# Attention, top-2 experts and a gated layer in one kernel: GpSimd's weight parts, VectorE's routing and a table are placed anew in the attention loop

## The reference, cut to what matters

```python
# q, k, v: 2 batches x 8 heads x 768 x 64; 4 sink keys, window of 128
scores = q @ k.T / sqrt(D), kept where key < n_sink or 0 <= query - key < window
a = exp(scores - max); a = a / (sum(a) + 1e-9)
x = a @ v                                            # 1536 tokens x 512
logits = x @ w_gate + log1p(exp(x @ w_noise)) * noise  # 8 experts
top2, weights = the two largest logits and their softmax
for each expert e: out += weight * (relu(x[mask] @ w1[e]) @ w2[e])   # 512 -> 1024 -> 512
h = out @ w_in                                       # 512 -> 2048
g = h * tanh(log1p(exp(h)))
result = g @ w_out                                   # 2048 -> 512
```

## Time and profile before

| | before |
|---|---|
| median of the runs (3) | 784.29 us (783.91 to 784.30) |
| the profiled execution's own time | 783.87 us |
| its span, first to last instruction | 781.8 us |
| TensorE busy | 760.9 us, 97% |
| VectorE busy | 515.4 us, 66% |
| GpSimd busy | 314.2 us, 40% |
| ScalarE busy | 285.4 us, 37% |

### The profile page before, as it was taken

One profiled execution on the slowest core, in us unless ns is written; L12 is line 12 of the kernel. 1 busy time (PEld: TensorE's weight loads), 2 busy tenths in 40 slices (PEclk: granted clock), 3 DMA queues, 4 the chain that ended last, 5 costly groups with the idle time before them and its releaser, 6 DMA issues.

```text
span 781.8 us, 13281 instructions
## 1 busy us (share of the span) xinstructions
PE 760.9 (97%) x4228; PEld 627.1 (80%) x4229; DVE 515.4 (66%) x905; ACT 285.4 (37%) x594; POOL 314.2 (40%) x331
## 2 busy tenths in 40 slices
PE   8999969999999999999999999989999999999997
PEld 5888757888888888888888888768888888888886
DVE  6789965545445454544545445468998888878876
ACT  6888713030303003030030300356555554545443
POOL 5599936673833708337083918511020020000000
PEclk9999979999999999999999999999999999999999
DMA  6475574644532615417153624010000110010001
GB/s 208 159 252 177 158 235 138 200 161 136 187 123 75 222 38 180 128 64 231 41 176 119 200 96 122 29 54 29 28 27 28 55 54 1 1 54 1 1 0 55
DMA packets 49486, 82.87 MB, mean 106 GB/s; under 512 B 18080, under 2 KB 22240, under 8 KB 49440
## 3 DMA queue, kind: packets, MB, share of 16 engines
q10 hardware_dynamic: 13600, 33.96, 13.2%
q1 hardware_dynamic: 31440, 33.89, 13.1%
q0 software_dynamic: 4400, 14.42, 6.6%
HBM read 66.01 MB, written 16.25 MB: 105 GB/s over the span
## 4 chain that ended last, share of the span: by engine, by line
PE 87%; DVE 6%; issue 3%; ACT 2%; POOL 1%; another core or an unknown queue 1%; DMA 0%; DVEq 0%; ACTq 0%; POOLq 0%
PE bank L1345 21%; PE bank L1356 21%; PE bank L1420 16%; PE bank L1401 15%; PE bank L1329 4%; PE bank L1235 2%; PE bank L1322 2%; PE bank L1210 2%; PE bank L1219 1%; PE bank L1244 1%; PE bank L1194 1%; PE bank L1393 1%; DVE x_sb L887 0%; DMA xg<-x_dram,first_idx 0%
## 5 line engine op out<-in xcount | busy, mean ns | idle before, releaser
L577 POOL TENSOR_TENSOR wgt<-stage,wgt 128x1024 f32 (+1 forms) x64 | 151.2, 2402 | 101.2 <-ACT wgt L738 101.2
L1356 PE MATMUL bank<-wgt,hT 128*128 (+1 forms) x744 | 185.3, 398 | 0.0
L1345 PE MATMUL bank<-wgt,xT 128*128 (+1 forms) x744 | 182.6, 394 | 0.0
L1345 PEld LDWEIGHTS bank<-wgt,xT 128*128 128x128 f32 x744 | 137.3, 188 | 27.5 <-DVE xT L1039 0.2
L738 ACT ACTIVATE wgt<-stage 128x1024 f32 (+1 forms) x64 | 61.6, 1045 | 265.0 <-PE bank L1356 252.0
L1356 PEld LDWEIGHTS bank<-wgt,hT 128*128 128x128 f32 x744 | 135.2, 188 | 25.3
L1420 PE MATMUL bank<-wgt,gT 128*128 128x512 f32 x576 | 141.3, 395 | 4.8 <-DVE gT L1137 4.8
L1401 PE MATMUL bank<-x2T,wgt 128*128 128x512 f32 (+1 forms) x588 | 138.1, 385 | 0.9 <-DVE x2T L1114 0.9
L1420 PEld LDWEIGHTS bank<-wgt,gT 128*128 128x128 f32 x576 | 108.4, 190 | 28.7 <-DVE gT L1137 6.1
L1401 PEld LDWEIGHTS bank<-x2T,wgt 128*128 128x128 f32 x588 | 108.6, 188 | 23.0 <-POOL wgt L651 1.1
L1083 DVE TENSOR_SCALAR h<-bank 128x512 f32<-128x512 f32 x62 | 42.9, 692 | 60.7 <-PE bank L1345 56.5
(11 more groups left out here) (174 smaller groups left out, 935.5 us busy)
## 6 DMA issues: line engine op xcount, KB each, us to landing
stage<-in_moe_w ACTq DMA_DIRECT2D x48, 512.0 KB, 3.4
stage<-in_moe_w SPq DMA_DIRECT2D x16, 512.0 KB, 5.4
y_dram<-y_sb SPq DMA_DIRECT2D x31, 256.0 KB
stage<-in_moe_w_in ACTq DMA_DIRECT2D x8, 512.0 KB, 4.0
stage<-in_moe_w_out ACTq DMA_DIRECT2D x8, 512.0 KB, 4.1
v_in<-in_v SPq DMA_DIRECT2D x8, 384.0 KB
x_dram<-x_sb SPq DMA_DIRECT2D x16, 192.0 KB, 2.7
out<-o_sb SPq DMA_DIRECT2D x12, 256.0 KB, 2.0
```

Of the source, the lines that this page charges most:

```text
L577: nc.gpsimd.tensor_tensor(cols(parity, 1, u * UNIT, UNIT), stage[:, u, :], cols(parity, 0, u * UNIT, UNIT).bitcast(fp32), ALU.subtract).th ...
L1345: ins = T.matmul(HA[half][:], xT[:, a, c, :], cols(par, b, c * F + half * 512, 512), start=c == 0 and n == 0, stop=c == NC - 1 and n == 2)
L1356: ins = T.matmul(YB[kk % 2][:], hT[:, a, c, :], cols(par, b, NC * UNIT + c * DM, DM), start=c == 0 and n == 0, stop=c == F // P - 1 and n ...
```

## The change

GpSimd's weight parts start at attention unit 10 and take five units to a weight unit, in the first, second and fourth of them. The table is a quarter as wide, is made in the pass of unit 42, and its readers repeat it by broadcast. VectorE's routing of batch 0 is spread over the passes of units 34 to 46. SP loads two weight units right after q and k and before it waits for the value matmuls.

```diff
--- before.py
+++ after.py
@@ -112,7 +112,7 @@
     xT_att = [attn.tensor(f"xT_att{i}", [P, 2, P], fp32) for i in range(2)]
     assert attn.at <= attn_end, (attn.at, attn_end)
     hot = Region(wgt_at + 2 * WCOLS * 4)
-    ramps = hot.tensor("ramps", [P, P, 2 * NT], f16)
+    ramps = hot.tensor("ramps", [P, P, QT], f16)
     row_hot = [hot.tensor(f"row_hot{i}", [P, P, NT], f16) for i in range(2)]
     assert hot.at <= wgt_at + 2 * WCOLS * 4 + 4 * (2 * S + 2 * QT * SEC)
 
@@ -261,7 +261,7 @@
         probs_ready = sem("probs_ready")
         probs_transposed = sem("probs_transposed")
         pT_ready = sem("pT_ready")
-        WEIGHTS_FROM = 14
+        WEIGHTS_FROM, WEIGHT_UNITS, WEIGHT_PARTS = 10, 5, (0, 1, 3)
         pT_cut = sem("pT_cut")
         pv_ready = sem("pv_ready")
         xT_copied = sem("xT_copied")
@@ -436,13 +436,12 @@
                 if i + 1 < NP:
                     sp.wait_ge(qk_ready, 4 * i)
                     load_qk(i + 1, (i + 1) % 2)
+                for u in range(2 * (i - 2), min(2 * (i - 1), UNITS)):
+                    src, to = unit_of(0, u)
+                    sp.dma_start(to, src).then_inc(unit_loaded[u], 16)
                 sp.wait_ge(pv_ready, QT * (i - 1))
                 load_v(i, i % 2)
                 store_x(i - 2)
-
-                for u in range(2 * (i - 2), min(2 * (i - 1), UNITS)):
-                    src, to = unit_of(0, u)
-                    sp.dma_start(to, src).then_inc(unit_loaded[u], 16)
 
                 if i == NP - 1:
                     sp.wait_ge(consts_ready, 1)
@@ -564,11 +563,12 @@
                     cut_probs(n - 1)
                     pad_sums(n - 2)
                 for u in (n, n + 1):
-                    if u >= WEIGHTS_FROM and (u - WEIGHTS_FROM) // 4 < UNITS and (u - WEIGHTS_FROM) % 4 < 3:
-                        first_set((u - WEIGHTS_FROM) // 4, (u - WEIGHTS_FROM) % 4)
-                if n == PROBS - 2:
+                    unit, part = (u - WEIGHTS_FROM) // WEIGHT_UNITS, (u - WEIGHTS_FROM) % WEIGHT_UNITS
+                    if 0 <= unit < UNITS and part in WEIGHT_PARTS:
+                        first_set(unit, WEIGHT_PARTS.index(part))
+                if n == PROBS - QT:
                     pool.wait_ge(qk_ready, 4 * NP)
-                    nc.gpsimd.tensor_copy(ramps[:], ramp[:].unsqueeze(2).broadcast_to([P, P, 2 * NT])).then_inc(ramps_ready, 1)
+                    nc.gpsimd.tensor_copy(ramps[:], ramp[:].unsqueeze(2).broadcast_to([P, P, QT])).then_inc(ramps_ready, 1)
 
             def remainders(s, parity):
                 for u in range(UNITS):
@@ -967,7 +967,7 @@
                     dve.wait_ge(ramps_ready, 1)
                 for w in range(2):
                     ms = slice(w * NT + g * QT, w * NT + (g + 1) * QT)
-                    V.tensor_tensor(row_hot[w][:, :, js], ramps[:, :, ms], r_h[:, ms].unsqueeze(1).broadcast_to([P, P, QT]),
+                    V.tensor_tensor(row_hot[w][:, :, js], ramps[:], r_h[:, ms].unsqueeze(1).broadcast_to([P, P, QT]),
                                     ALU.is_equal).then_inc(rows_ready, 1)
 
             V = nc.vector
@@ -990,19 +990,22 @@
                     qk_remainder(i + 1, t - 1)
                 if u == PROBS - 3 * QT:
                     gate_sums(0, 0, QT).then_inc(sums_ready, 1)
+                if u == PROBS - 2 * QT - 2:
+                    noisy_gates(0)
                 if u == PROBS - 2 * QT:
-                    noisy_gates(0)
                     pick_max(0, 0, rt3["lg"][:, 0:QT])
+                if u == PROBS - 2 * QT + 2:
                     pick_first(0, 0)
+                if u == PROBS - QT - 2:
+                    hide_best(0)
                 if u == PROBS - QT:
-                    hide_best(0)
                     pick_max(0, 1, by_token("cut"))
+                if u == PROBS - QT + 2:
                     pick_first(0, 1)
-                if u == PROBS - QT + 2:
+                    count_rows(0)
                     score_gap(0)
-                    count_rows(0)
+                if u == PROBS - 2:
                     first_expert(0)
-                if u == PROBS - 2:
                     rank_rows(0)
                 if u >= 6:
                     norm_step(u - 6, 2)
@@ -1052,7 +1055,8 @@
             after(V.tensor_reduce(rt["begin"][:], sel, AX.X, ALU.add))
             V.scalar_tensor_tensor(rt["p01"][:], rt["begin"][:], float(P), rt["p01"][:], ALU.mult, ALU.add)
             after(V.tensor_tensor(a_h[:], rt["begin"][:], a_u[:], ALU.add))
-            after(V.tensor_tensor(slot_hot[:], ramps[:, 0:32], a_h[:].unsqueeze(1).broadcast_to([P, 32, M]), ALU.is_equal))
+            after(V.tensor_tensor(slot_hot[:].rearrange("p t (g j) -> p t g j", j=QT), ramps[:, 0:32].unsqueeze(2).broadcast_to([P, 32, M // QT, QT]),
+                                  a_h[:].rearrange("p (g j) -> p g j", j=QT).unsqueeze(1).broadcast_to([P, 32, M // QT, QT]), ALU.is_equal))
             V.tensor_tensor(slot_hot[:], slot_hot[:], tok_h[:].unsqueeze(1).broadcast_to([P, 32, M]), ALU.mult).then_inc(hots_ready, 1)
             split_xT(0)
             dve.wait_ge(idx_summed, 1)
```

## The result

The changed kernel takes 779.79 us (median of 5, 779.3 to 780.8) against 784.30 for the kernel before beside it (median of 5, 783.91 to 785.7): a ratio of 0.994, 95% interval 0.9926 to 0.9954. The forecast was 780.3, with 779.0 to 782.8 as its range. The profiled execution of the changed kernel took 780.71 us with a span of 778.9, 0.9 us above the median.

A forecast was written before the change was run, and what follows sets the result against it. GpSimd's weight parts and VectorE's stretched instructions were taken to hold TensorE off pace in attention. Loop 4.35 - 0.8 = 3.55 plus table 0.4 gave 3.95 us off, so 780.3 us, range 779.0 to 782.8.

The forecast's parts named there:

- Which engine had lost the pace, and where: Attention loop: GpSimd, then VectorE, hold TensorE off its 10.96 us per pair from unit 24 on, losing 4.35 us.
- The step that GpSimd stops being the pace: Attention loop: with the new schedule ten units cost GpSimd 18.1 us against TensorE's 18.3.
- The step that single parts finish before the remainders begin: Attention passes: a single part ends 1.6 or 1.8 us after pass start, VectorE's remainders begin at 2.5 us.
- Two collisions: Attention loop: only two double parts still meet VectorE's remainders, each costing VectorE at most 1.09 us.
- 0.8 us left unrecovered: Of the loop's 4.35 us: 0.2 behind unit 20's collision, 0.4 for units 30 to 38, 0.2 for rank_rows.
- Batch 0's routing: VectorE, units 34 to 46: spreading it ends the bunching at unit 36; passes 34 and 38 exceed pace by at most 0.2 us.
- The table: End of attention: a quarter-size copy at unit 42 lets the last cuts come earlier; gain 0.4 us, bounds 0 and 1.0.
- The loads: SP queue: issuing two weight unit loads earlier, unit 0 at about 17 us, is worth nothing.
- rival 4: After attention: TensorE's clock rises too late for slot 0, making the kernel slower; 786.3 us at d = 12; chance 5%.
- Rival 1: Attention loop: VectorE's stretching stays and it keeps the pace, gain 2.7 us, 781.5 us; chance 25%.
- Rival 2: Slot 0's gather: the x stores' DMA backlog sets its start, gain 2.5 us, 781.8 us; chance 7%.
- Rival 3: Attention: the slower pairs come from something that stays, only the table's 0.4 and a little gained, 783.7 us; chance 8%.

The follow-up runs named there:

- parts_after: The kernel before with all GpSimd weight parts taken out of the attention loop and done behind it; 806.12 us in one execution.
- write_more: The kernel before, old schedule, weight parts replaced by memsets of 1260 and 1540 columns, expert 0's weights not prepared; 783.07 us in one execution.
- parts_only: The kernel before with only the new weight part schedule (units 10 to 48) and the earlier loads, old routing order and table; 0.996 of before.
- bunched: The changed kernel with the third part of each weight unit one attention unit earlier (first, second, third of five); 0.9965 of the kernel before.
- table_only: The kernel before with only the table a quarter as wide and made at unit 42; 1.0009 of before.
- norm_first: The changed kernel with the normalization of units 40 and 41 moved inside rank_rows; 0.9927 and, on the next chip, 0.9942 of the kernel before.
- routing_only: The kernel before with only VectorE's routing of batch 0 spread over units 34 to 46; 1.0001 of before.
- write_only: The kernel before, old schedule, weight parts replaced by memsets of 1024 and 1304 columns that read nothing, expert 0's weights not prepared; 0.9943 of before.
- loads_back: The changed kernel with SP's two weight unit loads behind the x store again; 1.0014 of the kernel before.

## Why the prediction was right, point by point

**Which engine had lost the pace, and where.** Right. The loss was 4.35 us by its count; parts_after and write_more put the attainable stretch at 66.38, so 4.20 were there to have.

**The weight parts.** Right in kind and size: 3.51 of 4.08 us (parts_only). The step that GpSimd stops being the pace was half of the argument, and the weaker half: write_more shows a GpSimd with the same busy share, longer parts and no loss. The step that single parts finish before the remainders begin was the one that counted; bunched undoes it for four weight units and loses 1.07 us. Two collisions of at most 1.09 us were counted, 2.2 together; the trace has 2.5 us of stretching, and the likeness of the sums is luck. Three remainders stand beside a subtraction and cost 0.32, 0.50 and 0.31 us, the first of them beside a single part (33.16), which by the prediction should have been done. The rest stands mainly in six remainders of 0.77 us instead of 0.56, each beside GpSimd's causal cuts, which the prediction did not count.

**0.8 us left unrecovered.** Too much: it was 0.31 in pair 36 and nothing in the others, so the loop gave 4.08, not 3.55. The table's term was too large by 0.30 in return, so the two terms together gave 4.18 where 3.95 stood. That the two errors offset each other is luck.

**Batch 0's routing.** Its share had been seen as VectorE's own overload at unit 36. It is 0.54 us alone, and the 2.04 us of pair 36 were nearly all stretching: with the old order they shrink to 0.26 in parts_only. What the old order still costs beside the new parts stands in the last pair, up to 0.62 us, where parts_only has TensorE wait 0.31 us for a normalization behind the second choice at unit 42; the table differs there too.

**The table.** The 0.4 us was the mis-sized term: 0.10 in the profiled pair, and table_only gives nothing. The next wait, the normalization behind rank_rows, was not in the sum; it grew from 0.20 to 0.56 us. What the prediction did not ask is what the table would cost if it were left: up to 1.35 us (18.26 against 16.91, the routing order differing as well).

**The loads.** "Worth nothing" was wrong as a statement on the edit: it carries the start at unit 10, and without it the kernel is 5.9 us slower in the loop and no faster than before. What the loads alone would do to the kernel before no run shows.

**What follows.** The 0.59 us between index and slot 0 had no step. The rows put them beside the clock: in the earlier trace rows the window's mean of 0.55 puts its rise at about 120.4, 5.9 us after the warming matmuls began at 114.54; after, the mean of 0.88 puts it at 115.1, 4.1 us after their start at 111.01, so less of the way is done at half speed. The prediction had written (rival 4) that the work before the rise moves as a block; it did, but the rise did not move with it. Nor is the 0.59 us clearly the change's. This interval has two values: 7.24 to 7.35 us in the kernel before, table_only and both of norm_first, and 6.68 to 6.89 in the nine others that have slot 0 right behind the index, parts_only and routing_only among them. What selects one was not tried. The 1.30 us at the end of the span have no step either. The windows of the gated layer's beginning show a longer time below full clock (by their means some 3.4 us at half speed, then 6.8), first before, then after:

```profile
520.00:525.00 5.00, 2.55 (x12) 1.77 (x10) 3.70 (x6) 3.09 (x6) 0.00 (x0) 1.00 0.00 0
525.00:530.00 5.00, 3.55 (x9) 2.78 (x10) 4.44 (x8) 3.03 (x6) 0.00 (x0) 0.66 0.00 0
```

```profile
520.00:525.00 5.00, 2.45 (x6) 1.97 (x7) 3.36 (x6) 3.08 (x6) 0.00 (x0) 0.63 0.00 0
525.00:530.00 5.00, 5.00 (x17) 3.98 (x16) 4.08 (x8) 3.06 (x5) 0.00 (x0) 0.69 0.01 3
```

From the first matmul of the gated layer to the end, nine of the 14 profiles of this study have 275.88 to 276.07 us, the kernel before and both of norm_first among them, and five have 276.84 to 277.53, both of the changed kernel among them. What selects the one or the other was not tried, and stays open; it is not part of what the change does to attention.

**The rivals.** Rival 1 (stretching stays, 781.5) falls: pairs 24 and 30 are at pace, the remainders went from 18.85 to 13.66 us. The Trainium skill (SBUF — State Buffer, Who interferes with whom) says that a VectorE instruction with two SBUF inputs contends with a GpSimd instruction that reads SBUF, and not with one that only writes it. write_only and write_more agree, with remainders of 0.53 to 0.66 us on the mean against 0.89 and 0.95. Of the prediction's two readings of that rule, the one as a matter of overlap is borne out, and the one as a toll on each part is not. Rival 2 (x stores) falls: the DMA engines were idle 2 us before the index. Rival 3 (no measurable change) falls: the ratio's interval excludes it. Rival 4 (the clock) falls: the clock was up 2.8 us ahead of slot 0; but loads_back shows what half clock costs in another place.

## What to carry to other kernels

When an engine is full and the loop behind it is late, test the fullness by itself: a stand-in of the same length that reads nothing costs one run, and here it cleared the busy share. Look then at how long the engine takes per unit too, since the stand-in changes that as well (7.44 against 7.97 us here). Where two engines' instructions stretch each other, look at where in the pass each one's stand before you take work away. An edit that gains nothing alone may be what carries another one; cost each edit both as added to the old kernel and as missing from the new one.

## What was not expected of the hardware

Memsets of 1540 columns (1.38 us) beside VectorE's remainders leave these at 0.53 to 0.58 us on the mean, while with the subtractions of 512 columns (1.28 us) in the kernel before the means are 0.89 and 0.95. The stretching goes both ways: where the remainder starts first (44.29 in the kernel before), the subtraction behind it, from 44.37, takes 1.59 us instead of 1.28. And one wait of 3.43 us on TensorE, in a loop that had run at full clock for over 20 us, brought half clock from about 35.2 us, within the wait, to about 42 us: the wait and what came of it cost 5.93 us together.
